# Moving query scaling and decay scans on VectorE in the first chunks of a fused attention, spectral-mixing and gated-MLP kernel

## What is computed

```python
# 1: linear attention with a decay per key dimension
for t in range(S):
    state = alpha[:, :, t, :, None] * state + np.einsum('bhd,bhe->bhde', k[:, :, t], v[:, :, t])
    y[:, :, t] = np.einsum('bhd,bhde->bhe', q[:, :, t], state)
x = y as (batch, seq, 384)
# 2: mixing over positions with angles from the data
theta = x @ w_theta
zr, zi = x * cos(theta), x * sin(theta)
u = x + einsum('ts,bsd->btd', w_tok_r, zr) + einsum('ts,bsd->btd', w_tok_i, zi)
x2 = u + np.maximum(u @ w_ch, 0.0)
# 3: gated MLP with mixing over positions
h = np.maximum(x2 @ w_in, 0.0); u, v = h[..., :512], h[..., 512:]
v_s = einsum('ts,bsd->btd', w_spatial, layernorm(v)) + b_spatial[None, :, None]
out = (u * v_s) @ w_out
```

## Time and profile before

| | us |
|---|---|
| median of 3 runs | 580.37 |
| profiled execution, own time | 581.29 |
| its span | 579.5 |
| TensorE busy (span share) | 566.0 (98%) |
| VectorE busy | 396.9 (68%) |
| ScalarE busy | 246.7 (43%) |
| GpSimd busy | 226.5 (39%) |

### The profile page before, as it was taken

How to read it: one execution, slowest core, us unless ns; L and a number is a source line. 1 busy time by engine, 2 the same in 40 slices (tenths; PEclk the granted TensorE clock), 3 DMA queues, 4 the chain that set the end, 5 groups by cost and what they waited for, 6 DMA issues and landing times.

```text
span 579.5 us, 13709 instructions
## 1 busy us (share of the span) xinstructions
PE 566.0 (98%) x5806; PEld 538.6 (93%) x5806; DVE 396.9 (68%) x626; ACT 246.7 (43%) x461; POOL 226.5 (39%) x184
## 2 busy tenths in 40 slices
PE   6899899999999999999999999999999999999997
PEld 5787799999999999999999989999999899989997
DVE  6988999788776766876544379978437852776253
ACT  2767555453544544545442226822432243134210
POOL 2356442442332522523422047463813481347131
PEclk9999999999999999999999999999999999999999
DMA  7952222232322332323033180200220022002002
GB/s 285 338 197 93 90 94 73 80 102 70 110 70 70 115 112 91 112 70 110 3 114 119 42 286 1 81 1 1 82 83 1 0 83 81 1 2 82 1 1 81
DMA packets 21229, 49.69 MB, mean 86 GB/s; under 512 B 1712, under 2 KB 16816, under 8 KB 20656
## 3 DMA queue, kind: packets, MB, share of 16 engines
q1 hardware_dynamic: 21168, 48.81, 24.2%
HBM read 39.37 MB, written 9.44 MB: 84 GB/s over the span
## 4 chain that ended last, share of the span: by engine, by line
PE 84%; DVE 9%; ACT 2%; POOL 2%; issue 1%; DMA 1%; DVEq 0%; ACTq 0%
PE psY L535 19%; PE psC L567 6%; PE psC L491 5%; PE psY L712 4%; PE psY L663 4%; PE psS L431 3%; PE psY L673 3%; PE psF L653 3%; PE psS L712 3%; PE psF L712 3%; PE psY L653 2%; PE psS L663 2%; PE psS L673 2%; PE psF L673 2%; PE psF L466 2%; PE psC L712 2%
## 5 line engine op out<-in xcount | busy, mean ns | idle before, releaser
L1381 POOL TENSOR_TENSOR z_lo<-cos_sin,z_hi 128x768 fp32r<-128x768 f32 x23 | 43.8, 1906 | 87.0 <-ACT z_hi L830 87.0
L1455 POOL TENSOR_TENSOR gated_lo<-raw_gated,gated_hi 128x384 fp32r<-128x384 f32 x32 | 35.9, 1126 | 70.4 <-ACT gated_hi L979 69.2
L1368 POOL TENSOR_TENSOR akq<-akq 128x512 f32<-128x512 f32 x23 | 27.3, 1188 | 70.7 <-DVE akq L1046 70.7
L1388 POOL TENSOR_TENSOR u_lo<-u_f,u_hi 128x384 fp32r<-128x384 f32 x24 | 29.2, 1245 | 46.1 <-ACT u_hi L835 46.1
L979 ACT ACTIVATE gated_hi<-raw_gated 128x384 fp32r<-128x384 f32 x32 | 16.4, 527 | 58.0 <-DVE raw_gated L1290 57.4
L535 PE MATMUL psY<-tok_r_hi,z_hi 128*128 128x384 f32 x117 | 41.0, 350 | 0.0
L1449 POOL TENSOR_TENSOR vn_lo<-raw_vn,vn_hi 128x512 fp32r<-128x512 f32 x24 | 33.7, 1423 | 17.0 <-ACT vn_hi L957 17.0
L535 PE MATMUL psY<-tok_i_hi,z_lo 128*128 128x384 f32 x117 | 39.2, 335 | 0.0
L535 PE MATMUL psY<-tok_i_lo,z_hi 128*128 128x384 f32 x117 | 39.2, 335 | 0.0
L535 PE MATMUL psY<-tok_r_hi,z_lo 128*128 128x384 f32 x117 | 39.2, 335 | 0.0
L535 PE MATMUL psY<-tok_i_hi,z_hi 128*128 128x384 f32 x117 | 39.1, 335 | 0.0
(11 more groups left out here) (309 smaller groups left out, 1839.6 us busy)
## 6 DMA issues: line engine op xcount, KB each, us to landing
akq<-akq SPq DMA_DIRECT2D x22, 770.0 KB, 4.5
v<-v_in SPq DMA_DIRECT2D x24, 192.0 KB, 4.6
x_dram<-u_f SPq DMA_DIRECT2D x8, 576.0 KB, 3.6
out<-ot SPq DMA_DIRECT2D x24, 192.0 KB, 1.9
raw_x<-x_dram SPq DMA_DIRECT2D x3, 1152.0 KB, 5.0
raw_tok_r<-w_tok_rT SPq DMA_DIRECT2D x6, 384.0 KB, 7.3
raw_tok_i<-w_tok_iT SPq DMA_DIRECT2D x6, 384.0 KB, 8.3
raw_sp<-w_spT SPq DMA_DIRECT2D x4, 576.0 KB, 6.2
```

Source lines behind the costliest of these rows:

```text
L1381: pool.tensor_tensor(Z[c][1][:], trigs[g % 2][:], f(Z[c][0][:]), ALU.subtract).then_inc(z_lo, 1)
L1455: pool.tensor_tensor(GA[1][:, j, half(h)], ug[:, j, half(h)], f(GA[0][:, j, half(h)]), ALU.subtract).then_inc(g_lo, 1)
```

## The change

Nothing is computed in another way; instructions move between engines and places.

- VectorE multiplies the queries of chunks 3, 4 and 5 (`own_queries`), right behind their second scan. GpSimd no longer does these three.
- VectorE scans the decays of chunks 4, 5 and 6 from the back at the end of slots 2, 3 and 4, behind the state and ahead of the z product. Before, it did so in the next slot, behind the mask.
- In slot 5 ScalarE rounds the weight parts 6 and 7 behind the sines, ahead of `z_high`, and then whole turns and the copy of the keys ahead of keeping xT. In slot 6 it copies x ahead of `z_high`, and in slot 5 x is copied without the two weight parts in front.
- VectorE does part 5 of the token weights in place of part 7 (`MID_SPLITS`), GpSimd part 7 in place of 5, behind z_lo of chunk 4.
- In slot 6 VectorE splits xT right behind the scan of chunk 7, ahead of the key product and the second scan.
- `channel_mix` waits for each low part of u when it needs it, no longer for all three ahead of the first.

```diff
-MID_SPLITS = (6, 7, 8, 9)
+MID_SPLITS = (5, 6, 8, 9)
+LOW_SPLITS = (0, 1, 2, 3, 4, 7, 10, 11)
...
+            def wait_tok(i):
+                if i in MID_SPLITS:
+                    pe.wait_ge(tok_lo_mid, MID_SPLITS.index(i) + 1)
+                else:
+                    pe.wait_ge(tok_lo, LOW_SPLITS.index(i) + 1)
...
-                    pe.wait_ge(tok_lo, s // 2 * 2 + 2)
+                    wait_tok(s // 2 * 2)
+                    wait_tok(s // 2 * 2 + 1)
...
-                pe.wait_ge(u_lo, (n // CT + 1) * CT)
...
                 for j in range(CT):
+                    if m_out == 0:
+                        pe.wait_ge(u_lo, n // CT * CT + j + 1)
...
-                if c == CHUNKS - 1:
-                    for i in SPLITS[c]:
-                        tok_high(i)
                 copy_x(c)
...
+                if c == CHUNKS - 1:
+                    for i in SPLITS[c]:
+                        tok_high(i)
                 if c > 1:
                     z_high(c - 1)
+                if c == CHUNKS - 1:
+                    whole_turns(c)
+                    copy_kT(c + 1)
                 if c:
                     keep_xT(c)
...
-                    if g < AHEAD:
+                    if g == CHUNKS:
+                        sines(g - 1)
+                        copy_x(g)
+                        z_high(g - 1)
+                    elif g < AHEAD:
...
+            def own_queries(g):
+                dve.wait_ge(decayed, g + 1)
+                s = akq_of(g)[0]
+                dve.tensor_tensor(Q[s], Q[s], ALPHA[s].rearrange("p (q t) -> p q t", q=PAIRS)[:, :, 0:P],
+                                  ALU.mult).then_inc(q_scaled, 1)
...
                 if c == CHUNKS - 1:
-                    decays_back(c + 1)
                     reduce_angle(c - 1)
...
+                if c == 2:
+                    decays_back(c + 1)
                 if c > 1:
-                    decay_keys(c + 1)
+                    scale_keys(c + 1)
                     decay_queries(c + 1)
+                    own_queries(c + 1)
                 reduce_angle(c - 1)
                 update_state(c)
+                if c > 1:
+                    decays_back(c + 2)
...
+                    if g == CHUNKS:
+                        reduce_angle(g - 1)
+                        mask_scores(g)
+                        multiply_z(g - 1)
+                        decays_back(g + 1)
+                        xT_low(g)
+                        scale_keys(g + 1)
+                        decay_queries(g + 1)
...
                 if c < CHUNKS - 1:
-                    scale_queries(c + 1)
                     z_low(c - 2)
             z_low(CHUNKS - 3)
-            tok_low(CHUNKS - 1)
             scale_queries(CHUNKS)
             z_low(CHUNKS - 2)
+            tok_low(CHUNKS + 1)
```

More of the change, by code:

```diff
@@ L522, in token_mix @@
                 if k < HALVES:
[L523 to L527, removed]
+                    wait_tok(k * CHUNKS + s // 2 * 2)
+                    wait_tok(k * CHUNKS + s // 2 * 2 + 1)
                 if h == 0:
@@ L1120, in _ @@
             decay_queries(0)
-            dve.wait_ge(decayed, 1)
-            dve.tensor_tensor(Q[0], Q[0], ALPHA[0].rearrange("p (q t) -> p q t", q=PAIRS)[:, :, 0:P],
-                              ALU.mult).then_inc(q_scaled, 1)
+            own_queries(0)
             decay_keys(1)
@@ L1168, in _ @@
                         make_x2(tile_of(b, c))
-                        xT_low(g)
+                        if g > CHUNKS:
+                            xT_low(g)
                         update_state(g)
```

## The result

| | before | with the change |
|---|---|---|
| median, us | 580.95 (580.19 to 581.88, 10 runs) | 583.93 (582.53 to 586.8, 10 runs) |
| profiled execution, us | 581.29 | 584.31 |
| its span | 579.5 | 582.1 |

The ratio of the times is 1.0053, with a 95% interval of 1.0036 to 1.0070: the change costs 3.1 us (2.1 to 4.1). The forecast was 2.3 more than before, 582.7, in a range of 579.8 to 584.8.

What follows compares the result with a forecast made beforehand. From 23 to 77 us VectorE's chain is as busy as TensorE, whose lateness at 77 us stays. A 5.4 us delay at slot 5 shrinks to 2.9; channel mix -0.6 gives +2.3: 582.7 us, range 579.8 to 584.8.

Steps and rivals of the forecast that it cites:

- slot 2: Chunk 2's stretch from one z product's end to the next: 2.65 us longer, from z_lo's turn, queries and added scan.
- slots 3 and 4: Stretches of chunks 3 and 4 between z product ends: each 1.38 us longer, 1.55 of it z_lo's turn.
- delay at slot 5: Lateness accumulated over slots 2 to 4 when slot 5 starts: 2.65 + 2 x 1.38 = 5.4 us.
- slots 5 and 6: Gains after slot 4: key product 1.2, xT copy behind angle rounding 0.37, two TensorE waits 1.0 us.
- channel mix: Waiting for low parts one by one in the last batch saves 0.6 us in all, between 0.3 and 0.7.
- The turn: Slots 2 to 4: GpSimd's z_lo slips between VectorE's key product and second scan, costing 1.55 us a slot.
- The queries: Query product moved to VectorE adds 0.73 us to its chain, three times, 2.2 us in all.
- The scan ahead of z: First scan moved behind the state takes 1.26, not 1.54 us, filling 0.89 idle; slot 2 gets +0.37.
- Behind slot 4: Slots 5 and 6: 1.2 us from the key product, 0.37 from the xT copy, 1.0 from TensorE's two waits.
- The load: akq's load lands 8.5 us after the z product, its scan asks at 8.56: 0 to 0.5 twice, taken as 0.
- The faster rival: VectorE keeps its place, z_lo goes behind the second scan: slots 3 and 4 are 9.15, total 578.0 us; chance 0.15.
- The slower rival: akq's load lands late (up to 0.5 twice), or the key product waits for z_lo too: 583.7 to 585 us; chance 0.1.

Runs made afterwards that it cites:

- mix_only: The kernel before with only the channel mix's three single waits added; 579.34 us, ratio 0.9982.
- change_again: The changed kernel itself, unaltered, measured and profiled a second time; 583.31 us.
- early: The changed kernel with the akq loads of chunks 5, 6 and 7 issued one slot earlier; 581.97 us, ratio 1.0035.
- hold_early: The changed kernel with the akq loads of chunks 5 to 7 one slot earlier and GpSimd's z_lo held until the second scan is done; 577.60 us, ratio 0.9959.
- own_q: The changed kernel with the first scans of chunks 5 to 7 back behind the mask, queries still on VectorE; 584.18 us, ratio 1.0071.
- own_q_hold: The changed kernel with first scans of chunks 5 to 7 back behind the mask and z_lo held until the second scan is done; 580.29 us, ratio 0.9992.
- x_only: The changed kernel without its two VectorE parts (query products, scans ahead of z); 577.74 us, ratio 0.9948.
- scan_only: The changed kernel with the three query products back on GpSimd, scans still ahead of z; 581.64 us, ratio 1.0011.
- hold_z: The changed kernel with GpSimd's z_lo in slots 2 to 4 also waiting for VectorE's second scan; 581.64 us, ratio 1.0018.

## Why the prediction was right

The direction, the mechanism and most terms were right. The figures in this table are differences to before (only the second scan's are durations), from the profile of the result, after its late start of 0.92.

| step | predicted | measured |
|---|---|---|
| slot 2 | +2.65 | +2.46 |
| slots 3 and 4, each | +1.38 | +1.23, +1.25 |
| second scan | about 2.8 | 2.66 |
| delay at slot 5 | 5.4 | 4.94 |
| slots 5 and 6 (1.2, 0.37, 1.0) | -2.6 | -2.55 (3.26 less mix_only's 0.71) |
| channel mix | -0.6 | -0.71 (mix_only; 1.0 by its medians) |
| sum | +2.3 | +1.7 in this profile; +2.9 in change_again's; +3.1 by the medians |

**The turn** was the right mechanism: three of three z_lo went ahead of the second scan. It was a little too dear. I had z_lo start only at the key product's end, 2.55 into the slot; it started at 2.44. That is why each of slots 3 and 4 is 0.14 shorter than worked out. The turn itself, where I had 1.55, is 1.36 a slot between early and hold_early (32.83 against 28.75), which differ in it alone, and 1.41 between own_q and own_q_hold.

**The queries** were right: 0.73 predicted, 0.74 measured (own_q_hold against x_only). **The scan ahead of z** was right too: the step from own_q_hold to hold_early is +0.37 in slot 2, the figure predicted, and -0.90 in each of slots 3 and 4. With both locks open this part is a gain of 1.4 in three slots. With the load in its old place it is none: scan_only, which has it without the queries, needs 31.54 for its slots where the kernel before needs 27.95.

**Behind slot 4** all terms held: -1.17 up to the z product of slot 5 (predicted 1.2), -0.37 more up to the mask of chunk 6 (0.37), and of the 1.72 behind it 1.0 is left for TensorE's two waits when the channel mix's 0.71 is taken off (1.0). x_only shows that they don't depend on the rest.

**The load** is the step that was mis-sized: "This is a tie: from 0 to 0.5 for each of two chunks. I take 0." It was indeed a tie, 0.0 in the first profile and 0.7 in the second, and I took the lower end of the range. In change_again the late load's 0.7 and the 0.55 of the rest, where the clock fell, make the step from +1.7 to +2.9, near the medians' +3.1; how much of the 0.55 is the clock's, and the shares over all executions, were not separated. That my +2.3 lies between the two profiles is in part luck: the turn was about 0.5 too dear over the three slots and the load up to 0.7 too cheap. More serious is what I did not draw from the tie. I compared the load with the scan that asks for it, once, and did not see that both ends hang on the z product, so that slot length and load form a loop of 10.5 us or more (the load's time and 6.0), under which no shorter VectorE chain could go.

**The faster rival** was therefore wrong as it stood, and half of its own sign would have spoken for it: hold_z's scans are 1.29, but its slots are not 9.2. It promised 578.0 with slots of 9.15 if only z_lo went behind the scan. hold_z did exactly that and ran 581.64, its slots at 10.6 to 10.9. With the load opened as well, hold_early ran 577.60 with slots of 9.16 and 9.17, and slot 2 longer by 1.1, both as the rival had them. The arithmetic of VectorE was right, and it was not the only thing that holds z. The slower rival's late load did occur, at the price given for it, but as part of the likeliest case and not in its place.

The best version is the change without its two VectorE parts: x_only, 577.74, or hold_early at 577.60; their ratios to before, 0.9948 and 0.9959, lie within each other's intervals, and x_only is the simpler. From the start of slot 2 on, x_only's span is the shorter (551.8 against 552.6), and so is its fastest time (576.66 against 577.39).

## What to carry to other kernels

Taking work off an engine also takes away the waits that it carried. GpSimd's query product had kept z_lo off VectorE's second scan, a service that no busy time or idle time shows, only the order of the rows: ask of each removed instruction what stood behind it in its list, and which instruction of the other engine that will now meet.

Moving a consumer one slot ahead moves its load's deadline ahead as well. Follow the load back to what frees its buffer: if that hangs on the instruction that now stands behind the consumer, load and slot form a loop, and its length is the floor for the slot. When two such floors are equal, removing either alone shows little or nothing (here 0.9 and 0.06 of 4.1 us); an experiment that opens one must be paired with one that opens both.

## What the runs showed of the hardware

A spell of half clock on TensorE can follow a gap of 1.6 us, and need not. In hold_z and scan_only the angle matmuls of slot 5 ran at a granted clock of 0.54 and 0.51 behind 1.61 and 1.91 us of idle time, for 1.3 and 1.4 us more. In the changed kernel gaps of 1.97, 1.07 and 1.58 us at the same matmuls were followed by a clock of 1.00:

```profile
37.81 0.44 PE L492 MATMUL psC<-theta_hi,xT_hi 128*128 128x384 f32 x1 [1.97 <-DVE xT_lo L1092]
...
58.91 0.44 PE L492 MATMUL psC<-theta_hi,xT_hi 128*128 128x384 f32 x1 [1.58 <-DVE xT_lo L1092]
```

In change_again it was 0.59 in the same slot (58 to 62 us), behind a gap of 1.79. In own_q it fell behind a gap of 1.60 in slot 3 and not behind one of 2.24 in slot 5. So the gaps that the locks make on TensorE carry a risk beyond their own length. What decides it, these runs leave open.

Slot 2 starts between 23.16 and 25.42 us with the same code ahead of it. VectorE's first key product, which the first loads release, starts between 5.01 and 5.72; most of the rest goes with the first sixteen score matmuls, which take 1.16 to 1.47 us in one group of executions and 2.08 in the other. For differences of 1 us in a kernel of 580 us this is the largest disturbance, and it is gone when slots are compared in place of spans.

A load of `akq`, 770 KB, took from 4.43 to 5.03 us in the slots that waited for it, and the slot grew and shrank with it.
